# First channel product of a transformer block: from single chunks and units to pairs of them with Strassen's seven products

## The reference, cut to what matters

```
x = moe(attention)                      # (4, 576, 512) -> 2304 rows of 512
mu, var = mean(x), mean((x - mu) ** 2)  # over the 512 features of a row
xn = (x - mu) / sqrt(var + 1e-6) * g_ln
ch = maximum(xn @ w_ch1, 0.0) @ w_ch2   # w_ch1 512 x 2048, w_ch2 2048 x 512
return x + ch
```

## Time and profile before

| | |
|---|---|
| median of 3 runs | 817.94 us (817.84 to 818.54) |
| the profiled execution, its own time | 820.35 us |
| its span, first to last instruction | 818.6 us |
| TensorE busy (matmul) in the span | 806.7 us |
| VectorE, ScalarE, GpSimd busy | 348.0, 301.2, 204.4 us |
| mean granted TensorE clock | 0.998 of full speed |

### The profile page before, as it was taken

One profiled execution on the slowest core, in us unless ns is written; L12 is line 12 of the kernel. 1 busy time (PEld: TensorE's weight loads), 2 busy tenths in 40 slices (PEclk: granted clock), 3 DMA queues, 4 the chain that ended last, 5 costly groups with the idle time before them and its releaser, 6 DMA issues.

```text
span 818.6 us, 13760 instructions
## 1 busy us (share of the span) xinstructions
PE 806.7 (99%) x5232; PEld 697.6 (85%) x5232; DVE 348.0 (43%) x773; ACT 301.2 (37%) x759; POOL 204.4 (25%) x296
## 2 busy tenths in 40 slices
PE   8999999999999999999999999999999999999998
PEld 6767888778887788889899999999989999999997
DVE  6876746375553845355753132231321313213111
ACT  5995675455554566345541111111111111111110
POOL 4885656332452434215520000000000000000000
PEclk9999999999999999999999999999999999999999
DMA  6453332311223210153530030030002003002001
GB/s 225 144 171 94 107 99 74 125 43 60 74 69 113 59 60 2 39 193 108 177 129 1 1 116 1 1 105 10 0 25 90 0 0 115 0 0 77 1 1 39
DMA packets 37750, 56.21 MB, mean 69 GB/s; under 512 B 2752, under 2 KB 20160, under 8 KB 37696
## 3 DMA queue, kind: packets, MB, share of 16 engines
q1 hardware_dynamic: 37696, 55.49, 20.6%
HBM read 46.04 MB, written 9.44 MB: 68 GB/s over the span
## 4 chain that ended last, share of the span: by engine, by line
PE 84%; DVE 6%; ACT 4%; issue 3%; POOL 1%; ACTq 0%; POOLq 0%; DVEq 0%
PE psum L1129 23%; PE psum L1131 23%; PE psum L1130 23%; PE psum L1050 5%; PE psum L1095 4%; ACT probs L649 3%; DVE neg_max L851 2%; PE psum L1110 2%; PE psum L1115 2%; PE psum L1212 1%; DVE mix_buf L926 1%; POOL unit_raw L612 1%; PE psum L1181 1%; DVE vn_r L895 0%; DVE row_sum L859 0%
## 5 line engine op out<-in xcount | busy, mean ns | idle before, releaser
L1021 DVE SCALAR_TENSOR_TENSOR h_r<-psum,h_r 128x384 fp32r<-128x384 f32 x96 | 53.5, 557 | 287.2 <-ACT h_r L814 287.2
L814 ACT ACTIVATE h_r<-psum 128x384 fp32r<-128x384 f32 x96 | 47.2, 492 | 340.5 <-PE psum L1131 340.5
L1129 PE MATMUL psum<-xn_r,units_r 128*128 128x384 f32 x384 | 129.6, 337 | 0.0
L1131 PE MATMUL psum<-xn_r,units_r 128*128 128x384 f32 x384 | 129.4, 337 | 0.0
L1130 PE MATMUL psum<-xn_r,units_r 128*128 128x384 f32 x384 | 128.9, 336 | 0.0
L545 POOL TENSOR_SCALAR probs<-probs,row_inv 128x512 f32<-128x512 f32 (+4 forms) x160 | 93.0, 597 | 110.6 <-DVE row_inv L864 110.6
L1131 PE MATMUL psum<-units_r,h_r 128*128 128x512 f32 x288 | 113.7, 395 | 0.0
L1130 PE MATMUL psum<-units_r,h_r 128*128 128x512 f32 x288 | 113.5, 394 | 0.0
L1129 PE MATMUL psum<-units_r,h_r 128*128 128x512 f32 x288 | 111.9, 389 | 0.0
L649 ACT ACTIVATE probs<-psum,neg_max 128x512 f32<-128x512 f32 (+4 forms) x160 | 90.0, 567 | 46.9 <-DVE neg_max L851 44.7
L851 DVE TENSOR_REDUCE neg_max<-psum 128x1 f32<-128x512 f32 (+4 forms) x160 | 80.7, 538 | 60.9 <-PE psum L1050 59.7
(11 more groups left out here) (107 smaller groups left out, 1407.9 us busy)
## 6 DMA issues: line engine op xcount, KB each, us to landing
qk_raw<-qk SPq DMA_DIRECT2D x32, 576.0 KB, 4.0
unit_raw<-w_ch SPq DMA_DIRECT2D x32, 256.0 KB, 3.2
y_norm<-y_scratch SPq DMA_DIRECT2D x6, 768.0 KB, 6.3
y_res<-y_scratch SPq DMA_DIRECT2D x6, 768.0 KB, 4.6
out<-y_res SPq DMA_DIRECT2D x18, 256.0 KB, 2.1
v_raw<-vN SPq DMA_DIRECT2D x16, 256.0 KB, 2.8
y_scratch<-mix_buf SPq DMA_DIRECT2D x16, 256.0 KB, 2.0
w_raw<-w_in SPq DMA_DIRECT2D x8, 256.0 KB, 4.6
```

Of the source, the lines that this page charges most:

```text
L814: act.activation(h_hi[:, f % HR, :], h_bank[:, f % 2, 0:CHUNK], ACT.Relu).then_inc(h_hi_done, 1)
L1021: dve.scalar_tensor_tensor(h_lo[:, f % HR, :], h_bank[:, f % 2, 0:CHUNK], 0.0, h_hi[:, f % HR, :].bitcast(F32), ALU.max, ALU.subtract).the ...
L1129: pe.matmul(dst, a_hi, b_hi, start=start, stop=False)
L1131: return pe.matmul(dst, a_lo, b_hi, start=False, stop=stop)
```

## The change

The rows are now taken as 3 pairs of chunks (768 rows), the hidden features as 8 blocks of two units, and the 512 input features as two halves. A pair and a block thus form a 2 x 2 by 2 x 2 product of parts (a part of the product has 384 rows and 128 features, and each factor part has two 128-deep steps). Strassen's method gives the four results C11, C12, C21, C22 with seven products M1 to M7 instead of eight:

- GpSimd makes four sums of weight parts for each block once (`combine_weights`). The weights are not scaled any more; g goes onto the transposed rows (`tile_drain`, VectorE, PSUM to `raw_x`).
- For each pair four sums of row parts are made (`combine_x`, GpSimd, one of the first pair's on VectorE), and all seven operands of 128 x 768 are split once a pair (`operand_hi` on ScalarE, `operand_lo` on VectorE).
- For each product the weight operand (128 x 256) is split anew: `product_hi` (ScalarE) and `product_lo` (GpSimd), three products ahead, four slots. The second product's weights are split anew for each block (`second_hi`, `second_lo`, 128 x 512 twice).
- Each product is 2 x 3 matmuls of 384 columns into one of two banks. ScalarE keeps M1 in SBUF (`keep_m1`). VectorE forms C11 to C22 with nine additions of a bank and a buffer (`sum_to`). ScalarE and VectorE then split the four results from SBUF (`hidden_hi`, `hidden_lo`).
- The second product of a block comes in twelve pieces (`piece`, three matmuls of 512 columns), two behind each of the first six products of the next block. It accumulates in six banks, of which each takes a row tile of the pair.
- The next pair's row tiles are normalised one at a time, one a block in the first six blocks, and each is transposed between M2 and M4 of the block after.
- The last mixer's five w groups stand between the products of the very first block. The first pair's six tiles are normalised, transposed, combined and split during the last mixer's u and s groups.
- The loops over chunks are written out.

```diff
+        M1, M7, M2, M4, M6, M5, M3 = range(7)
+        W_SUM, C11_SUM, V_SUM, C21_SUM, U2_SUM, U3_SUM, U4_SUM, C22_SUM, C12_SUM = range(1, 10)
+        ORDERS = [[M1, M2, M3, M7, M5, M6, M4]] + [[M1, M7, M2, M4, M6, M5, M3]] * (PAIRS - 1)
+        LN0 = U0 - 1
+        LO0 = S0 + 2
+        XT_AT = [U0 + 5, U0 + 6, U0 + 7, U0 + 7, S0, S0 + 1]
+        PIECES_IN = [2, 2, 2, 2, 2, 2, 0]
+        TAIL = [0, 1, 2, 6, 7, 8, 3, 9, 4, 10, 5, 11]
+        W_GROUPS_AT = [[0], [1], [], [2], [3], [4], []]
...
@@ block.gpsimd
+            for g in range(W0):
                 mixer_read(B - 1, g)
                 if is_kind(g, "s"):
                     mixer_finish(B - 1, g)
...
+                if g in (S0 + 1, S0 + 2, S0 + 4):
+                    combine_x(0, (S0 + 1, S0 + 2, S0 + 4).index(g))
+                if g >= W0 - 3:
+                    product_lo(g - W0 + 3)
+            for i in range(NB):
+                p, q = i // BLOCKS, i % BLOCKS
+                for j in range(7):
+                    if p == 0 and q + 1 < BLOCKS and j in (0, 1, 2, 3):
+                        combine_weights(q + 1, j)
+                    if 7 * i + j + 3 < 7 * NB:
+                        product_lo(7 * i + j + 3)
+                    if j == 3:
+                        second_lo(i, 0)
+                    elif j == 6:
+                        second_lo(i, 1)
+                    elif j == 4 and tile_of(i) is not None:
+                        tile_rstd(tile_of(i))
+                    if next_pair(i) is not None:
+                        if q == BLOCKS - 2 and j in (4, 6):
+                            combine_x(next_pair(i), j // 2 - 2)
+                        if q == BLOCKS - 1 and j in (1, 2):
+                            combine_x(next_pair(i), 1 + j)
...
@@ block.scalar
+                for j in range(7):
+                    if i == 0:
+                        for m in W_GROUPS_AT[j]:
+                            mixer_read(B - 1, W0 + m)
+                    if i >= 1 and j == 0:
+                        hidden_hi(i - 1, C12)
+                    if 7 * i + j + 3 < 7 * NB:
+                        product_hi(7 * i + j + 3)
+                    if next_pair(i) is not None and q == BLOCKS - 1 and j >= 1:
+                        operand_hi(next_pair(i), j - 1)
+                    if q == 0 and p >= 1 and j == 0:
+                        operand_hi(p, 6)
+                    if j == M1:
+                        keep_m1(i)
+                    elif j == M2:
+                        hidden_hi(i, C11)
+                    elif j == M4:
+                        second_hi(i, 0)
+                    elif j == M6:
+                        hidden_hi(i, C21)
+                    elif j == M5:
+                        hidden_hi(i, C22)
+                    elif j == M3:
+                        second_hi(i, 1)
...
@@ block.vector
+            def sum_to(dst, i, j, other, needs=None):
+                dve.wait_ge(m_done, 7 * i + j + 1)
+                if needs is not None:
+                    dve.wait_ge(c_summed, SUMS * i + needs)
+                dve.tensor_tensor(dst, product_bank(i, j), other, ALU.add).then_inc(c_summed, 1)
...
+                for j in range(7):
+                    if j == M1 and i >= 1:
+                        sum_to(c_raw[C12], i - 1, M3, u2_buf, U4_SUM)
+                        hidden_lo(i - 1, C12)
+                        if q == 0:
+                            operand_lo(p, 6)
+                        if q == 1 and p >= 1:
+                            for m in range(CT, PT):
+                                add_out(p - 1, m, 6 + m + 1)
+                    elif j == M7:
+                        dve.wait_ge(m1_kept, i + 1)
+                        sum_to(u3_buf, i, M7, m1_buf)
+                    elif j == M2:
+                        sum_to(c_raw[C11], i, M2, m1_buf)
+                        hidden_lo(i, C11)
+                        if tile_of(i) is not None:
+                            tile_stats(tile_of(i))
+                    elif j == M4:
+                        if tile_through(i) is not None:
+                            tile_drain(tile_through(i), product_bank(i, TILE))
+                        sum_to(v_buf, i, M4, u3_buf, W_SUM)
+                    elif j == M6:
+                        sum_to(c_raw[C21], i, M6, v_buf, V_SUM)
+                        sum_to(u2_buf, i, M6, m1_buf)
+                        sum_to(u3_buf, i, M6, u3_buf)
+                        hidden_lo(i, C21)
+                    elif j == M5:
+                        sum_to(u2_buf, i, M5, u2_buf, U2_SUM)
+                        sum_to(c_raw[C22], i, M5, u3_buf, U3_SUM)
+                        if q == 0 and p >= 1:
+                            for m in range(CT):
+                                add_out(p - 1, m, 6 + m + 1)
+                        hidden_lo(i, C22)
+                        if tile_of(i) is not None:
+                            tile_normalise(tile_of(i))
+                    if next_pair(i) is not None and q == BLOCKS - 1 and j >= 1:
+                        operand_lo(next_pair(i), j - 1)
...
@@ block.tensor
+            def product(i, j):
+                n, p, q = 7 * i + j, i // BLOCKS, i % BLOCKS
+                pe.wait_ge(wp_lo_done, n + 1)
+                if q == 0:
+                    pe.wait_ge(xn_lo_done, 7 * (p + 1) if p == 0 else 7 * p + j + 1)
+                bank_read(pe, i, j)
+                bank = product_bank(i, j)
+                for k in range(2):
+                    last = three(bank, wp_hi[:, n % WP, k, :], wp_lo[:, n % WP, k, :], xn_hi[j][:, k, :],
+                                 xn_lo[j][:, k, :], k == 0, k == 1)
+                last.then_inc(m_done, 1)
...
+            for i in range(NB):
+                r = 0
+                for j in range(7):
+                    if j == M4 and tile_through(i) is not None:
+                        bank_read(pe, i, TILE)
+                        transpose_xn(tile_through(i), product_bank(i, TILE))
+                    if i == 0:
+                        for m in W_GROUPS_AT[j]:
+                            mixer(B - 1, W0 + m)
+                    product(i, j)
+                    if i >= 1:
+                        for _ in range(PIECES_IN[j]):
+                            piece(i - 1, r)
+                            r += 1
+            for r in TAIL:
+                piece(NB - 1, r)
```

More of the change, by code:

```diff
@@ L144, in transformer_block @@
[L144 to L150, removed]
+        WP = 4
+        raw_x = place("raw_x", KD * 2 * CHUNK, F32, 0).rearrange("p (k n) -> p k n", k=KD)
@@ new lines, in transformer_block @@
+        h_r = place("h_r", 4 * 2 * CHUNK, F32R).rearrange("p (c a n) -> p c a n", c=4, a=2)
+        h_hi, h_lo = h_r[:, :, 0], h_r[:, :, 1]
+        for j in (M6, M4):
+            operands[j] = place(f"operand{j}", 4 * CHUNK, F32R).rearrange("p (a k n) -> p a k n", a=2, k=2)
+        xn_hi = [operands[j][:, 0] for j in range(7)]
+        xn_lo = [operands[j][:, 1] for j in range(7)]
+        AFTER_U_END = at[0]
+        blocks = [block0] + [place(f"block{b}", BLOCK_COLS) for b in range(1, BLOCKS)]
@@ L508, in _ @@
+            for b in range(AFTER_S, AFTER_W):
+                load_block(b)
             for s in range(2):
                 sp.wait_ge(y_stored[s], stored_by(s, nth_y(B, 0)))
[L510 to L523, removed]
@@ L829, in _ @@
+            hidden_hi(NB - 1, C12)
         @block.vector
@@ L1004, in _ @@
+            dve.wait_ge(misc_loaded, 16)
+            for g in range(W0):
                 if is_kind(g - 2, "v"):
@@ L1043, in _ @@
+            sum_to(c_raw[C12], NB - 1, M3, u2_buf, U4_SUM)
+            hidden_lo(NB - 1, C12)
+            for m in range(PT):
+                add_out(PAIRS - 1, m, TAIL.index(6 + m) + 1)
         @block.tensor
@@ L1221, in hidden @@
-            def hidden(c, f, first):
-                if first:
-                    pe.wait_ge(u_lo_done, f + 1)
-                if f == 0:
-                    pe.wait_ge(xn_lo_done, CT * (c + 1))
-                if not (first and f < 2):
-                    pe.wait_ge(h_lo_done, FU * c + f - 1)
-                for k in range(KD):
-                    last = three(h_bank[:, f % 2, 0:CHUNK], ch1_hi[f][:, k, :], ch1_lo[f][:, k, :], xn_hi[:, k, :],
-                                 xn_lo[:, k, :], k == 0, k == KD - 1)
-                last.then_inc(h_made, 1)
@@ L1247, in chunk @@
-            def chunk(c, first, last):
-                for f in range(FU):
-                    hidden(c, f, first)
-                    if f >= 2:
-                        output(c, f - 2, first)
-                    if f == FU - 2 and not last:
-                        if first:
-                            pe.wait_ge(copied, nth_copy(B, 0))
-                        transpose_xn(c + 1)
-                output(c, FU - 2, first)
-                output(c, FU - 1, first)
-            chunk(0, True, False)
```

503 lines of the change are left out of this document (300 added, 203 removed).

## The result

The changed kernel takes 809.77 us (median of 4, 809.39 to 812.33) against 817.93: ratio 0.9905 (95% interval 0.9884 to 0.9926), 8.2 us less. A second batch gave 809.58 against 817.97, 0.9896 (0.9881 to 0.991). The forecast was 799.5, range 793 to 808: the sign is right, the gain less than half of the 18.4 forecast, the time 1.8 us outside the range. The profiled execution has a span of 807.8 us, 10.8 under that of before.

A forecast was written before the change was run, and what follows sets the result against it. TensorE was taken to bound the kernel: number of matmuls times their distance, until another engine is late. The terms -25.0 - 1.3 + 1.4 + 1.1 + 3.4 + 2.0 gave -18.4, so 799.5 us from 817.94, range 793 to 808.

The forecast's parts named there:

- 144 matmuls, -25.0: First product on TensorE: 1008 matmuls in place of 1152, at 0.1735 us each, 25.0 us less.
- The two waits of before, -1.3: TensorE's waits for the first transposes and a u group disappear: 0.6 and about 0.7, 1.3 us less.
- Switching +1.4: TensorE changing between 384- and 512-column matmuls, some 285 times against 192: 0 to 2.8 us more, taken as 1.4.
- single transposes +1.1: Row tiles transposed one at a time on TensorE: 0.50 us against 0.44 each, 1.1 us more over 18 tiles.
- The common block at 0: Ordinary block, 15.6 us on TensorE or 16.1 with a tile: other engines stay covered, at a price of 0.
- C12's chain: VectorE and ScalarE steps up to C12, which frees M3's bank for the next M7: slack 0.2 to 0.8 us.
- Pair boundaries, 3.4 (0.6 to 6): Blocks around the two pair changes: operand splits delay C12 (1.2 us), residual adds C22's split (0.5), twice: 3.4 us more.
- The port read as a full lock: VectorE and GpSimd excluding each other for whole SBUF instructions: the boundary block would cost 4 us a boundary.
- the overlap of 0.6 us in the earlier trace: VectorE and GpSimd operations overlapping before the change: read as the trace agreeing with a lock in size but not wholly.
- The first block, 2.0 (0.5 to 4): Ahead of the first M1, TensorE waits until all seven operands are split: 0.5 to 4 us, taken as 2.0.
- the stretched port: Rival, 20%: the shared port lengthens boundaries, first block and tile blocks; about 813.5 us at worst, 806 to 808 with half.
- All is hidden: Rival, 17%: boundaries and first block cost 1 us together, switches nothing; 24.2 us less, 793.7 us.

The follow-up runs named there:

- Experiment 9: Against the kernel of experiment 8, M3's six matmuls are issued twice in each block, 144 more matmuls: 816.76 us, 0.9983 of the kernel before the change.
- experiment 1: Against the changed kernel, GpSimd's low parts in blocks 7 and 15 cut to one or two columns, leaving out computation: 801.69 us, 0.98 of the kernel before.
- experiment 6: Against the changed kernel, the first three products' weights split in the last mixer's u groups, not its last s groups: 810.21 us, 0.9914 of the kernel before.
- Experiment 3: Against the changed kernel, each first-block product waits for its own operand's low part, not all seven: 805.83 us, 0.9849 of the kernel before.
- experiment 4: Against the changed kernel, thirteen needless 128-column matmuls put ahead of M1's wait in the first block: 808.75 us, 0.9886 of the kernel before.
- experiment 8: Changed kernel with splits deferred past pair boundaries, own-operand waits in the first block, earlier first weights and residual adds spread: 794.07 us, 0.9709 of the kernel before.

## Why the prediction was wrong

Point by point, in its own steps:

- **144 matmuls, -25.0.** Right: 25.2 at the measured distances, and 23.0 for the same number put back, waits included.
- **The two waits of before, -1.3.** Right; neither is in the trace after.
- **Switching +1.4, single transposes +1.1.** Too much: together they came to some 0.3. Experiment 9's trace has as many matmuls of either kind as the one before, half again as many switches and no wait for a sum: summed from start to start, its 1152 of 384 columns and 863 of 512 take 401.15 us, those of before 401.25. So more switches cost nothing that these sums would show. A single transposed tile takes 0.35 us and delays the matmul behind it by 0.11: 0.46, against the 0.50 forecast and 0.44 before.
- **The common block at 0.** Right: 16.1 us with a tile and 15.6 without, both as forecast, without idle time. The slack of 0.2 to 0.8 on C12's chain held, but for 0.3 us in block 1.
- **Pair boundaries, 3.4 (0.6 to 6).** This is the step that failed: 8.3 us of waits. The six splits were priced at 0.95 us each, which is what they cost undisturbed (experiment 1), and of the 0 to 2.3 us by which C12 might be late the sum took 1.2. Beside GpSimd five of the six took 1.5 to 2.4. And the path was incomplete: C12's sum, which frees M7's bank, was the only one taken to be late in the last block; the others had 1 us or more in the common block and were not followed here. In the trace C22's sum, which frees M1's bank, is late as well and costs 2.0 us at each boundary. The rows had shown the stretch: 1.30 for 0.68. The sum used it for one rival only and left it out of its central term.

  The port read as a full lock, the Trainium skill's reading ("SBUF — State Buffer", "SBUF: two separate sides"), came nearer here: its estimate of 4 us a boundary stands against 4.5 and 3.0 of waits on M1 and M7 (4.5 at both without the clock), and in the trace after, each long split ended 0.8 us after the GpSimd operation that it met (experiment 1). The prediction took the overlap of 0.6 us in the earlier trace rows for a sign against a full lock. But that pairs the split with the GpSimd operation that began after it. The one under way when it began, at 389.98, ended at 390.73:

```profile
389.75 0.98 POOL L565 TENSOR_TENSOR x_r<-mix_buf,x_r 128x288 fp32r<-128x288 f32 x1 [0.76 <-ACT x_r L701]
```

  The split ended 0.55 us after that, and GpSimd's next took 1.48 in place of 1.04: a record's length includes the waiting.
- **The first block, 2.0 (0.5 to 4).** Measured 3.2, within its bounds, with row sums of up to 2.56 us on GpSimd and splits of up to 2.23 on VectorE. By experiment 6 the chain counts and not GpSimd's total. Experiment 3 shows that 2.3 of the 3.2 came from waiting for all seven operands where M1 wants one.
- **No term for the clock.** Missing altogether: 4.5 us in the ledger, some 3 of them real. The granted clock was 1.00 throughout the late stages of before, in which no wait of TensorE reached 1 us. Both the boundaries and the first block pay, and experiment 4 shows for the latter that idleness is the cause.

From the -18.4 of the sum to the ledger: boundaries +4.9, clock +4.5, first block +1.2, an s group and block 1 +0.9, switching and transposes -2.5, matmuls -0.3.

Of the rivals, the stretched port was the one that came true, at a time somewhat above its 806 to 808. Its parts came out otherwise, so that the nearness is partly luck: it had 9.4 us for the boundaries (8.3, and the clock on top), 4 for the first block (3.2) and 6 for the blocks with a tile, which waited for nothing. "All is hidden", 793.7, is what order and narrower waits give: experiment 8 at 794.07, with the computation whole. So the expected gain was there to be had; the changed kernel gave it back at two boundaries and one start.

What stays open: 0.7 us between the ledger and the two traces; why a wait of 2.0 us brought the clock down at once at some boundaries (the second of the changed kernel, both of experiment 3) and not at others (the first of the changed kernel), and why even 2.5 us more did not at the first of experiment 6. No run here separates these.

## What to carry to other kernels

When VectorE operations with two SBUF inputs are put beside GpSimd work, price them at 1.5 to 2.5 times what they take alone (here 0.95 us became 1.49 to 2.42 for five of six), and look at what stands behind them on VectorE: if it is a read that frees a PSUM bank, order it first and the splits that are due later behind it. On a kernel in which TensorE is never idle, allow 1.5 us on top of a new wait of 2 to 3 us, for the clock; a wait for another engine that comes soon behind it takes that back, as at the second boundary here. And ask for each wait whether it names the one thing needed: waiting for all seven operands where one was wanted cost 3.9 us with its clock.

## What the runs showed of the hardware

The stretch of 768-column splits was larger than expected: 0.95 us alone, 1.54 in the mean over the changed kernel, up to 2.42, each long one at the boundary ending 0.8 us after the GpSimd operation that it met. GpSimd's operations of the same size went from 1.85 to 2.56. VectorE's sums with one input in PSUM kept 0.55 throughout. Half-clock stretches came after waits of 2.0 to 3.2 us, though not after every one (none after 2.0 and 2.5 at experiment 6's first boundary), and lasted about 3.4 us, once 6.9. A filler of needless matmuls kept the clock up but did not shorten the wait: 1.0 us gained, against 3.9 for removing most of it.
